# Products of ones in every mLSTM unit, and an earlier decay product

## The reference

```
C = np.zeros((B, H, D, D)); n = np.zeros((B, H, D)); m = np.full((B, H), -1e+30)
for t in range(S):
    m_new = np.maximum(f_gate[:, :, t] + m, i_gate[:, :, t])
    f_stab = np.exp(f_gate[:, :, t] + m - m_new)
    i_stab = np.exp(i_gate[:, :, t] - m_new)
    C = f_stab * C + i_stab * np.einsum('bhd,bhe->bhde', vt, kt)
    n = f_stab * n + i_stab * kt
    h_tilde = np.einsum('bhde,bhe->bhd', C, qt)
    denom = np.maximum(np.abs(np.einsum('bhd,bhd->bh', n, qt)), 1.0)
    y[:, :, t] = h_tilde / denom / (1.0 + np.exp(-o_gate[:, :, t]))
x = y as (1536, 320)
p = domain_probs / (domain_probs.sum(-1, keepdims=True) + 1e-09)
for e in range(4):
    out += p[:, e:e + 1] * (np.maximum(x @ w1[e], 0.0) @ w2[e])
a = out @ w_a; b = out @ w_b
return (a * b) @ w_out
```

## Time and profile before

| | |
|---|---|
| median of the runs | 673.39 us |
| profiled execution | 672.74 us |
| its span | 671.0 us |
| TensorE busy | 660.2 us, 98% of the span |
| mean granted clock of TensorE | 0.924 of full speed |
| DVE, ACT, POOL busy | 204.8, 195.3, 175.0 us |
| transfers | 31.04 MB, 46 GB/s over the span |

### The profile page before, as it was taken

How to read it: one execution, slowest core, us unless ns; L and a number is a source line. 1 busy time by engine, 2 the same in 40 slices (tenths; PEclk the granted TensorE clock), 3 DMA queues, 4 the chain that set the end, 5 groups by cost and what they waited for, 6 DMA issues and landing times.

```text
span 671.0 us, 9410 instructions
## 1 busy us (share of the span) xinstructions
PE 660.2 (98%) x3793; PEld 593.2 (88%) x3793; DVE 204.8 (31%) x421; ACT 195.3 (29%) x407; POOL 175.0 (26%) x194
## 2 busy tenths in 40 slices
PE   6999999999999999999999999999999999999998
PEld 5888989898998998998998998999888888888887
DVE  6454555422232231312312232332222221122212
ACT  4334343411233111331122321324233332332221
POOL 3232244500143000430004400023223632364221
PEclk9655555899999999999999999999999999999999
DMA  4244332220002200032000310000400040000002
GB/s 129 88 164 132 96 113 69 95 80 1 0 1 95 79 0 1 1 94 79 1 1 1 94 40 1 1 0 19 115 1 0 1 104 30 1 1 0 28 13 78
DMA packets 23002, 31.04 MB, mean 46 GB/s; under 512 B 1968, under 2 KB 18896, under 8 KB 22960
## 3 DMA queue, kind: packets, MB, share of 16 engines
q1 hardware_dynamic: 21296, 27.52, 13.4%
q10 hardware_dynamic: 1664, 2.93, 1.6%
HBM read 28.25 MB, written 1.97 MB: 45 GB/s over the span
## 4 chain that ended last, share of the span: by engine, by line
PE 96%; DVE 2%; POOL 0%; ACT 0%; DMA 0%; issue 0%; ACTq 0%; DVEq 0%; POOLq 0%
PE PS L905 12%; PE PS L906 12%; PE PS L958 11%; PE PS L957 11%; PE PS L956 11%; PE PS L907 11%; PE PS L908 6%; PE PS L909 6%; PE PS L871 6%; PE PS L827 3%; PE PS L841 2%; PE PS L816 2%; PE PS L794 1%; PE PS L856 1%; PE PS L795 1%; PE PS L801 0%
## 5 line engine op out<-in xcount | busy, mean ns | idle before, releaser
L958 PE MATMUL PS<-w2h,hl 128*128 128x320 f32 x528 | 163.2, 309 | 0.0
L956 PE MATMUL PS<-w2h,hh 128*128 128x320 f32 x528 | 162.7, 308 | 0.3 <-POOL w2l L395 0.3
L957 PE MATMUL PS<-w2l,hh 128*128 128x320 f32 x528 | 163.0, 309 | 0.0
L735 DVE SCALAR_TENSOR_TENSOR hl<-PS,hh 128x512 fp32r<-128x512 f32 x96 | 66.4, 692 | 238.2 <-ACT hh L476 238.2
L905 PE MATMUL PS<-xt,w1h 128*128 128x512 f32 x336 | 133.7, 398 | 0.0
L906 PE MATMUL PS<-xt,w1h 128*128 128x512 f32 x336 | 132.7, 395 | 0.0
L907 PE MATMUL PS<-xt,w1l 128*128 128x512 f32 x336 | 131.4, 391 | 0.0
L476 ACT ACTIVATE hh<-PS 128x512 fp32r<-128x512 f32 x96 | 57.5, 599 | 224.4 <-PE PS L909 224.4
L377 POOL TENSOR_TENSOR w1l<-s,w1h 128x384 fp32r<-128x384 f32 x56 | 56.4, 1016 | 246.5 <-ACT w1h L465 246.5
L956 PEld LDWEIGHTS PS<-w2h,hh 128*128 128x128 f32 x528 | 99.1, 188 | 5.7 <-issue 0.7
L957 PEld LDWEIGHTS PS<-w2l,hh 128*128 128x128 f32 x528 | 99.1, 188 | 4.9
(11 more groups left out here) (111 smaller groups left out, 551.7 us busy)
## 6 DMA issues: line engine op xcount, KB each, us to landing
kvo<-in_tok SPq DMA_DIRECT2D x12, 480.0 KB, 4.7
qk<-in_qk_t SPq DMA_DIRECT2D x24, 160.0 KB
s<-in_w SPq DMA_DIRECT2D x3, 1280.0 KB, 6.2
s<-in_w SPq DMA_DIRECT2D x3, 1024.0 KB, 5.5
s<-in_w_out SPq DMA_DIRECT2D x3, 640.0 KB, 5.1
out_y<-acc SPq DMA_DIRECT2D x12, 160.0 KB, 1.9
s<-in_w SPq DMA_DIRECT2D x6, 256.0 KB, 6.4
s<-in_w_a SPq DMA_DIRECT2D x6, 256.0 KB, 3.2
```

The costliest lines, as they stand in the source:

```text
L735: nc.vector.scalar_tensor_tensor(out=hl[:, k % RING, :], in0=PS[:, k % L1_BANKS, :], scalar=0.0, in1=f32(hh[:, k % RING, :]), op0=ALU.max, ...
L956: nc.tensor.matmul(bank, high, w2h[:, j, :], start=(j == 0), stop=False)
L957: nc.tensor.matmul(bank, high, w2l[:, j, :], start=False, stop=False)
L958: nc.tensor.matmul(bank, low, w2h[:, j, :], start=False, stop=(j == slices_of(st) - 1)).then_inc(l2_done, 1)
```

## The change

`outputs(u)` gets two products of ones ahead of its own, for u = 1 to 9; they go to the bank of the outputs, columns 384 to 511, which nothing reads. The 12 products at the start become 14, the 6 behind the second decay product 20, and the 5 in the first turn go. The decay product of unit 2 moves from the end of TensorE's first turn to a place behind the scores of unit 1. On ACT the exponentials of unit 2 move ahead of those of the turned logs; on POOL the mask of unit 2 moves ahead of the gating of unit 0. The state product moves from column 256 to column 192 of its banks, which leaves columns 384 to 511 free in all of them.

```diff
--- before.py
+++ after.py
@@ -65,7 +65,7 @@
 
         PS = ctx.enter_context(nc.psum_tensor("PS", [P, 8, 512], F32))
         DEC, SCORE, INTER, UPD, OUT, XPOSE = 0, 2, 4, 5, 6, 7
-        OLD_COLS = 256
+        OLD_COLS, BUSY_COLS = 192, 384
         L1_BANKS, YT_BANK, L2_BANK = 3, 3, 4
 
 
@@ -380,11 +380,9 @@
             for u in range(NU):
                 if u < OLD:
                     update_keys(u)
-                if u == 1:
-                    gate_output(0)
                 if u + 1 < NU:
                     clear_later(u + 1)
-                if u >= 2:
+                if u >= 1:
                     gate_output(u - 1)
                 for k in first_slices(u):
                     split_w1(0, k)
@@ -524,12 +522,13 @@
             for u in range(1, NU):
                 if u == 1:
                     gates_of(1)
+                if u + 1 < NU:
+                    weights(u + 1)
+                if u == 1:
                     act.wait_ge(ex_turned, 2)
                     nc.scalar.activation(ex[:, :, :, :].rearrange("p a c h -> p (a c h)"), PS[:, XPOSE, BH:BH + 2 * REST], ACT.Exp).then_inc(ex_ready, 1)
                     o = BH + 2 * REST
                     nc.scalar.activation(ex_state[:, :, :, :].rearrange("p c b a -> p (c b a)"), PS[:, XPOSE, o:o + REST // 2], ACT.Exp).then_inc(ex_ready, 1)
-                if u + 1 < NU:
-                    weights(u + 1)
                 if u >= 2:
                     x_high(u - 2)
                     gates_of(u)
@@ -794,11 +793,11 @@
                     nc.tensor.transpose(PS[:, bank, k * P:(k + 1) * P], src[:, k * P:(k + 1) * P], identf[:, :])
                 return nc.tensor.transpose(PS[0:64, bank, 2 * P:3 * P], src[:, 2 * P:DM], identf[:, :])
 
-            def keep_busy(n):
+            def keep_busy(n, bank=INTER):
 
                 pe.wait_ge(pool_const, 4)
                 for _ in range(n):
-                    nc.tensor.matmul(PS[:, INTER, 0:P], ones[:, :], ones[:, :], start=True, stop=True)
+                    nc.tensor.matmul(PS[:, bank, BUSY_COLS:BUSY_COLS + P], ones[:, :], ones[:, :], start=True, stop=True)
 
             def log_weights(u):
 
@@ -864,6 +863,7 @@
                 pe.wait_ge(pool_const, 7)
                 if u >= 1:
                     pe.wait_ge(num_ready, u)
+                    keep_busy(2 if u < NU - 2 else 0, OUT)
                 for q in range(2):
                     pe.wait_ge(p_ready, 2 * u + q + 1)
                     for p in range(NP):
@@ -965,17 +965,19 @@
                     pe.wait_ge(xlo_ready, 2 * NU)
                 transpose(YT_BANK, acc[:, u, :]).then_inc(yt_done, 1)
 
-            keep_busy(12)
+            keep_busy(14)
             products(0)
             keep_busy(6)
             log_weights(0)
             turn_first_logs()
             log_weights(1)
-            keep_busy(6)
+            keep_busy(20)
             for u in range(1, NU):
                 if 1 < u < NU - 1:
                     log_weights(u + 1)
                 products(u)
+                if u == 1:
+                    log_weights(2)
                 if u >= B:
                     from_state(u)
                     x_transpose(u - 2)
@@ -984,9 +986,6 @@
                     turn_rest_logs()
                 if u - 1 < OLD:
                     update(u - 1)
-                if u == 1:
-                    keep_busy(5)
-                    log_weights(2)
             l1(0)
             outputs(NU - 1)
             l1(1)
```

## The result

The kernel with the change takes **670.04 us** (median of 11 runs, 661.7 to 681.25), the kernel before 674.32 us (median of 11, 672.73 to 677.03). The ratio is 0.9859, interval 0.9817 to 0.9901; it leaves out runs more than 1.5% above their kernel's fastest, which here are the executions in which the clock stayed low longest, so where such runs occur the text goes by the medians of all runs. The forecast was 632.

The account below looks back on a forecast made before the run. It took TensorE's own time at 1.2 GHz in the mLSTM stage as the bound. Terms -6.05, -29.4, -3.7, -3.4 and +1.0 sum to -41.6 from 672.74, with 0.65 for the median: 632 us, range 628 to 677.

Parts of the forecast that it names:

- The wait and the move: Before the first weighing: 14 more ones fit inside the 3.50 us wait at no cost; moved decay product waits 0.1 us.
- the clock holds: Whole mLSTM stage: the clock stays at 2.4 GHz, giving 632 us, bounds 628 to 640; chance 0.55.
- the sum's term for the start: Up to the outputs of unit 1: they start at 25.55 us against 31.60, a change of -6.05 us.
- that for eight units: Outputs of unit 1 to those of unit 9: units take 5.86 us in place of 9.53, together -29.4 us.
- two ones are 0.46 of 5.86 us, which may be too little or just enough: In the units: doubt whether two products of ones per unit hold the clock, given with the midway fall, chance 0.12.
- Wherever it was kept or raised, products of ones had just run: Trace of the kernel before: ones preceded every stretch where the clock held or rose; being busy did neither.
- The rival: Between scores of units 1 and 2: clock falls and stays low, eight pairs cost +6.9 us, 677 to 678; chance 0.28.
- Its other case: Start: the clock is lost already at 17.3 us, so the start gains nothing, 680 to 681 us; chance 0.07.
- Nothing later would raise the clock: In the units: two ones in 10.4 us are too few to bring the clock back, so units stay at half clock.
- the midway rival: In the units: the clock holds for some, then falls; 656 us for the middle, 640 to 672 overall; chance 0.12.
- The sum for a clock that holds: Start, units, last outputs and first expert: terms add to -41.6 us at full clock, giving 632 us.
- The other engine as the bound: In the units: clock holds, but DVE or a unit's loads stretch units to 7 us, 642 us; chance 0.05.

Follow-up runs that it names:

- experiment 5: Changed kernel plus four products of ones ahead of the outputs of unit 0 and three ahead of the scores of unit 2: median 676.54 us of four runs.
- experiment 2: Changed kernel without the two products of ones ahead of the outputs of units 1 to 9; the filled wait stays: median 665.12 us of four runs.
- experiment 3: Changed kernel with 12 and 6 products of ones at the start in place of 14 and 20, so the wait is idle again: 679.87 us, ratio 1.0106.
- experiment 1: Changed kernel with four products of ones ahead of the outputs of units 1 to 9 in place of two: median 663.73 us of four runs.
- experiment 10: Changed kernel with four products of ones ahead of every unit's outputs through unit 9, two ahead of the scores of unit 2: median 658.42 us.
- experiment 6: Changed kernel with two products of ones ahead of the outputs and two ahead of the scores of units, four ahead of outputs 0: median 636.41 us.
- experiment 9: As experiment 7, but the products of ones inside the units have 41 columns in place of 128: 695.34 us, ratio 1.0331.
- experiment 11: Experiment 6 plus six products of ones in the row-transfer wait and 23 in place of 20 in the weighing wait: 635.58 us, ratio 0.9437.
- experiment 7: As experiment 6, with three products of ones in place of each two of the units: 640.07 us, ratio 0.9498.
- experiment 4: Changed kernel with only the decay product's move: 12 and 6 products of ones at the start, five in the first turn, none in units: median 670.37 us.

## Why the prediction was wrong, step by step

- **The wait and the move were right.** The 20 products fill the wait (0.68 us left), and the moved decay product waits for no transfer (0.1 us was forecast; 0.20 in experiment 5).
- **The step that failed is the likeliest case itself**, "the clock holds", at 0.55. In every execution of the change it was lost, for 71 to 116 us. In the profiled one the sum's term for the start is -1.75 us in place of -6.05, and that for eight units +6.9 in place of -29.4. The rows of before told that ones raise the clock and that a busy engine does not. They did not tell how many are enough, and "two ones are 0.46 of 5.86 us, which may be too little or just enough" should have carried the weight that it did not get. Experiments 2, 3 and 5 show no gain from two in one place; 1 and 10 that four in one place help for part of the units; 6 that two and two hold it in three runs of four.
- **A reading too narrow.** "Wherever it was kept or raised, products of ones had just run" holds up to 119 us only. In the kernel before the clock came back at 123.1, behind eight first-layer products of 512 columns, and stayed full to the end without any ones. That pointed to long products, which experiment 9 then showed to matter.
- **The rival's place and price were right for the executions at its end.** Fall around the first outputs (forecast: between the scores of units 1 and 2; measured 20.4 and 21.1), outputs of unit 1 at 29.85 (29.2), unit 10.39 (10.39), a pair 0.86 (0.86), 677 to 678 (677.8 to 679.07, and 681.25). Its other case, the clock lost before the scores of unit 1, said 680 to 681; experiment 3, where it is lost at 13.85, has 679.87. Of the 0.65 us too much in 29.85, 0.30 is the scores' later start (17.96 for 17.66).
- **"Nothing later would raise the clock" held for two ones a unit as far as the profiles show** (the change twice, experiments 3 and 5), and not for four: experiment 1 regains it twice inside the units. Four of the change's eleven runs have 71 us at half clock; whether they lost it later or regained it is open, for none was profiled. For their time the midway rival's sum serves: 661.8 is inside its 640 to 672, and its middle, 656, is too low by 6. It had 0.12, and of eleven runs seven lie in its bounds.
- **One outcome for a kernel was the wrong frame.** The chances stood for my ignorance of one answer; each execution gives its own. The forecast of a median over such runs should have been one of a mixture, between 662 and 678. The range of 628 to 677 took most of that in; 632 did not.
- **The sum for a clock that holds was good, though it decided nothing here.** The runs' line gives 630 at no half clock, the sum said 632. Experiment 11 checks it apart from that line: 635.58 us with 44 ones around the units where the change has 18; less 26 x 0.23 = 6.0 it is 629.6. Its units, 6.16 less 0.46 for two ones, are 5.70 (forecast 5.66 of TensorE's own, 5.86 with waits), and its outputs of unit 1, at 26.87 less 1.38 for six more ones, are at 25.5 (forecast 25.55). One reading in the sum is slightly off: of the 6.79 us from the outputs of unit 10 to those of unit 11 the outputs are 3.28, since the first layer starts at 119.63, not 3.40; it moves the sum by under 0.1.
- **The other engine as the bound** (0.05) did not come: 0.3 us of wait for DVE in all of experiment 11, 0.5 in experiment 5's full-clock units. It shows most with four ones in one place, 2.6 us in experiment 10, where a unit with such a wait takes 6.61 us for 6.18.

The section "HAM oscillation — how this bites in real kernels" of "TensorE: Matmul & The Clock Gate" in the Trainium skill puts the loss down to idle gaps between bursts. The kernel before agrees with it (idle from 14.2 to 17.2, then half clock), and the falls in experiments 6 and 10 agree in kind, at the end of waits of 1.81 and 0.91 us, though the gaps that the page speaks of are longer. Experiment 9 does not agree: its clock falls at 22.0, ten microseconds behind its last wait of 0.38, and stays at half for 122.70 us with no gap at all. By that rule alone experiments 7 and 9 would have taken the same time; they are 55 us apart.

## What to carry to other kernels

Where a stage is busy throughout and still at 1.2 GHz, filling idle time was not enough in this kernel: put long products (128 columns here) among the short ones, spread through the unit, look whether they also fill waits, and take only as many as hold the clock, since each is paid for, and at 1.2 GHz about twice (0.43 us for 0.23). Read the mean clock of every run, not the time alone: a median over executions that lose the clock at different places hides what the kernel can do. Half a dose can be worth no more than none, as experiment 2 shows beside the change: measure none, half and double, each in one place and in two.

## What the runs showed of the hardware that was not expected

- The same kernel spent from 71 to 116 us at 1.2 GHz, in steps that repeat (four runs at 71, two at 92, three at 110). What decides in which unit the clock goes is open; the profiles show the place and no event that is unique to it. The nearest is a wait for DVE of 0.25 to 0.91 us, which stands at all four losses inside the units and also, without a loss, in most turns of experiment 10.
- The clock came back inside units with four ones, at 31.6 and 86.2 us in experiment 1, and in experiment 6 behind the 20 ones, at 15.4. In no profile with two ones a unit or none did it come back between the outputs of unit 1 and the first layer.
- At the wait ahead of the second decay product, which ends at about 12 us, or within 2 us behind it the clock fell in the five profiles where the wait was 1.28 us (experiment 10), 1.45 (7), 1.51 (3), 1.75 (4) and 1.81 (6), and not where it was 1.47 (before) or between 0 and 1.17 (the other seven). On TensorE experiment 3 runs the same products as the kernel before up to there, so the same work can keep the clock or lose it. Behind the 20 ones it came back each time (experiments 6, 7 and 10), behind six it did not (3 and 4).
- A product of 41 columns takes 0.20 us where one of 128 takes 0.23, and did not keep the clock: 695.34 us against 640.07.
